# Windowed attention, MLP and routed experts in one kernel: the attention's tail reordered around MLP step 0, x of block 0 split from PSUM, filler matmuls from unit 10 on

## The reference, cut to what matters

```python
def _attn_ref(q, k, v, mem_k, mem_v):          # B=4, H=8, S=768, D=64, 8 memory keys
    for c in range(nc):                        # chunks of 32 queries
        k_full = np.concatenate([mem_k, k_ctx], axis=2)   # 16 keys to the left, 8 to the right
        scores = scale * np.matmul(q_c, k_full.transpose(0, 1, 3, 2))
        scores = scores - np.max(scores, axis=-1, keepdims=True)
        a = np.exp(scores)
        a = a / (np.sum(a, axis=-1, keepdims=True) + 1e-09)
        out[:, :, c_start:c_end] = np.matmul(a, v_full)

def _moe_ref(x, w_in, w_out, a, b):            # x 3072x512, w_in 512x2048, w_out 2048x512
    h = x @ w_in
    P = a[0] + a[1] * h + a[2] * h**2 + a[3] * h**3
    Q = 1.0 + np.abs(b[0]) * np.abs(h) + np.abs(b[1]) * h**2
    return (P / (Q + 1e-6)) @ w_out

def _moe2_ref(x, w_gate, w1, w2):              # 8 experts, each token goes to its best one
    ...
```

## Time and profile before

| | |
|---|---|
| three runs, median (lowest to highest) | 1076.66 us (1076.14 to 1079.69) |
| profiled execution | 1077.24 us |
| its span in the profile | 1075.4 us |
| mean granted TensorE clock | 0.976 of full speed |
| PE busy | 1013.0 us, 94% |
| DVE busy | 673.4 us, 63% |
| ACT busy | 589.9 us, 55% |
| POOL busy | 385.7 us, 36% |
| chain that ended last, by engine | PE 80%, DVE 8%, ACT 6%, issue 3%, DMA 2%, POOL 1% |

### The profile page before, as it was taken

The page is one execution under the profiler, slowest core; times in us unless marked ns, Lnnn a source line. Parts: engine busy times, 40 slices in busy tenths (PEclk is TensorE's granted clock), DMA queues, the critical chain, the costliest instruction groups (busy, mean ns, idle before and its releaser), DMA issues.

```text
span 1075.4 us, 20448 instructions
## 1 busy us (share of the span) xinstructions
PE 1013.0 (94%) x6272; PEld 834.9 (78%) x6273; DVE 673.4 (63%) x1327; ACT 589.9 (55%) x1256; POOL 385.7 (36%) x367
## 2 busy tenths in 40 slices
PE   8888889999999999999999999739999999999996
PEld 5767778888888888888888878527888888888885
DVE  6776788768867977887797778655225254322221
ACT  7876788766676666667667656605215144212121
POOL 2575344443444444344334434421212222212111
PEclk9998899999999999999999999959999999999999
DMA  8999500100010001001000120218115141111100
GB/s 315 386 407 353 221 1 21 33 27 20 0 59 0 20 0 59 20 0 59 0 20 1 40 98 1 99 59 303 32 46 186 46 185 33 42 40 34 49 24 14
DMA packets 34142, 90.05 MB, mean 84 GB/s; under 512 B 4262, under 2 KB 10534, under 8 KB 34096
## 3 DMA queue, kind: packets, MB, share of 16 engines
q1 hardware_dynamic: 29536, 76.86, 19.6%
q0 software_dynamic: 4560, 12.59, 3.5%
HBM read 72.13 MB, written 19.66 MB: 85 GB/s over the span
## 4 chain that ended last, share of the span: by engine, by line
PE 80%; DVE 8%; ACT 6%; issue 3%; DMA 2%; POOL 1%; DVEq 0%; POOLq 0%; ACTq 0%; SPq 0%
PE PS L478 22%; PE PS L573 21%; PE PS L671 14%; PE PS L705 14%; ACT prob L745 2%; PE PS L691 2%; PE PS L597 2%; PE PS L529 1%; PE PS L656 1%; DMA attention_out_t<-out_t 1%; DVE PS L910 1%; PE PS L500 1%; PE PS L609 1%; DVE g_sb L964 1%; DVE den L959 1%
## 5 line engine op out<-in xcount | busy, mean ns | idle before, releaser
L478 PE MATMUL PS<-xs,weights 128*128 (+1 forms) x1152 | 287.9, 399 | 0.0
L478 PEld LDWEIGHTS PS<-xs,weights 128*128 128x128 f32 x1152 | 215.5, 190 | 44.2
L573 PE MATMUL PS<-weights,g_hi 128*128 128x512 f32 x768 | 238.0, 391 | 6.1 <-POOL g_lo L1222 3.2
L1222 POOL TENSOR_TENSOR g_lo<-g_sb,g_hi 128x512 fp32r<-128x512 f32 x96 | 124.5, 1297 | 331.1 <-ACT g_hi L792 323.6
L573 PEld LDWEIGHTS PS<-weights,g_hi 128*128 128x128 f32 x768 | 143.5, 188 | 39.1 <-POOL g_lo L1222 6.3
L573 PE MATMUL PS<-weights,g_lo 128*128 128x512 f32 x384 | 149.6, 389 | 0.0
L671 PE MATMUL PS<-weights,xg_hi 128*128 x448 | 141.8, 398 | 3.1 <-DVE xg_lo L1155 2.6
L775 ACT ACTIVATE b_ln<-PS,cf 128x512 f32<-128x512 f32 x96 | 66.1, 689 | 128.2 <-PE PS L478 128.2
L705 PE MATMUL PS<-weights,h_hi 128*128 x432 | 135.8, 395 | 0.7 <-DVE weights L1032 0.7
L1225 POOL TENSOR_TENSOR den<-den,b_r 128x512 f32<-128x512 f32 x96 | 124.2, 1294 | 6.0 <-ACT b_r L798 6.0
L1155 DVE TENSOR_TENSOR xg_lo<-PS,xg_hi 128x512 fp32r<-128x512 f32 x29 | 20.0, 690 | 141.9 <-ACT xg_hi L815 141.9
(11 more groups left out here) (206 smaller groups left out, 1634.6 us busy)
## 6 DMA issues: line engine op xcount, KB each, us to landing
e_raw<-w_exp SPq DMA_DIRECT2D x35, 512.0 KB, 6.5
qk<-qk_all SPq DMA_DIRECT2D x32, 480.0 KB, 8.3
vw<-v_all SPq DMA_DIRECT2D x32, 384.0 KB, 8.0
w_raw<-w_mlp SPq DMA_DIRECT2D x16, 512.0 KB, 8.9
attention_out_t<-out_t SPq DMA_DIRECT2D x16, 384.0 KB, 7.2
x_raw<-attention_out_t SPq DMA_DIRECT2D x12, 512.0 KB, 5.0
mlp_out<-x SPq DMA_DIRECT2D x6, 1024.0 KB, 5.1
x_raw<-w_exp SPq DMA_DIRECT2D x5, 512.0 KB, 3.4
```

The costliest lines, as they stand in the source:

```text
L478: last = pe.matmul(PS[:, H_BANK + f % 2, :], w[:, wp], rhs, start=k == 0, stop=k == 3 * KT - 1)
L573: last = pe.matmul(PS[:, ACC_BANK + s, :], gp[:, f % 2, s * P:(s + 1) * P], w[:, wp], start=f == 0 and k == 0, stop=f == FT - 1 and k == 2)
L1222: pool.tensor_tensor(g_lo[:, q], g_sb[:], g_hi[:, q].bitcast(F32), ALU.subtract).then_inc(g_lo_done, 1)
```

## The change

1. *x of block 0 from PSUM.* For units 0 to 7 ACT writes the part of the output that belongs to the first 512 tokens directly into `xs` as `hi`: all 384 columns of an even unit, 128 of an odd one. The remaining 256 columns of the odd unit go to `out_t` as before. DVE subtracts `hi` from the PSUM bank to get `lo` (`lower_first`). PE's V of unit `u` waits for that (`first_lo_done`) as well, since both use the bank. The stores of pairs 0 to 3 shrink from 768 to 256 columns, the two loads of x for block 0 and POOL's four splits are gone.
2. *Weights.* POOL splits five pieces, after units 9, 13, 17, 21 and 25, where it split four after 11, 15, 21 and 27. Each load and each split in the steps moves accordingly; the piece that was split in step 7 is now split in step 6.
3. *Seam.* H of step 0 moves to iteration 31, H of step 1 to iteration 34. DVE does both of its last copies of transposed probabilities in step 0, ACT copies outputs 28 and 29 in step 0 and 30 and 31 in step 1. L580 moves from step 0 to step 4.
4. *Fillers.* From unit 10 on PE issues one matmul on zeros (128x384) ahead of each V.
5. The splits of x for the later blocks stand in steps 8, 10, 12 and 14, where they stood in 6, 8, 10 and 12.

```diff
-W_LOAD = {8: (0,), 12: (1,), 18: (2,), 22: (3,), 28: (4,), 30: (5,), 31: (6, 7), 32: (8, 9), 33: (10, 11), 34: (12, 13), 35: (14, 15)}
-W_POOL = {11: 0, 15: 1, 21: 2, 27: 3}
-W_STEP = {0: 4, 1: 5, 2: 6, 3: 7, 4: 8, 5: 9, 6: 10, 7: 11, 8: 12, 9: 13, 11: 14, 13: 15}
+W_LOAD = {6: (0,), 10: (1,), 14: (2,), 18: (3,), 22: (4,), 29: (5,), 30: (6,), 31: (7, 8), 32: (9, 10), 33: (11, 12), 34: (13, 14),
+          35: (15,)}
+W_POOL = {9: 0, 13: 1, 17: 2, 21: 3, 25: 4}
+W_STEP = {0: 5, 1: 6, 2: 7, 3: 8, 4: 9, 5: 10, 6: 11, 7: 12, 9: 13, 11: 14, 13: 15}
-H_EARLY = {32: 0, 33: 1}
+H_EARLY = {31: 0, 34: 1}
+STEADY_FROM = 10
+DIRECT = 8
-STEADY = 0
+STEADY = 1
...
+        def copies(u):
+
+            return (u + 1) // 2 if u < DIRECT else u + 1 - DIRECT // 2
...
@@ PE, unit loop
                     if u >= 2:
-                        pe.wait_ge(out_t_copied, u - 1)
-                    warm(STEADY, 6 + u % 2)
+                        if u - 2 < DIRECT:
+                            pe.wait_ge(first_lo_done, u - 1)
+                        if u > 2:
+                            pe.wait_ge(out_t_copied, copies(u - 2))
+                    if u >= STEADY_FROM:
+                        warm(STEADY, 6 + u % 2)
...
@@ ACT, copy_out
+                p, lo, hi = u // 2, (u % 2) * HALF, (u % 2 + 1) * HALF
                 act.wait_ge(out_t_ready, u + 1)
+                if u < DIRECT:
+                    act.activation(xs[:, p, lo:min(hi, TB)], PS[:, 6 + u % 2, 0:min(hi, TB) - lo], ACT.Copy).then_inc(first_hi_done, 1)
+                    if u % 2 == 0:
+                        return
+                    lo = TB
...
@@ DVE
+            def lower_first(u):
+
+                at = slice((u % 2) * HALF, min((u % 2 + 1) * HALF, TB))
+                dve.wait_ge(first_hi_done, u + 1)
+                if u % 2:
+                    dve.wait_ge(out_t_copied, copies(u))
+                dve.tensor_tensor(xs[:, KT + u // 2, at], PS[:, 6 + u % 2, 0:at.stop - at.start],
+                                  xs[:, u // 2, at].bitcast(F32), ALU.subtract).then_inc(first_lo_done, 1)
...
                 if d >= T_LAG:
                     copy_prob_t(d - T_LAG)
+                if 0 <= d - O_LAG < DIRECT:
+                    lower_first(d - O_LAG)
...
@@ DVE, step 0
-                if st.in_period(0) and st.m < 2:
-                    copy_prob_t(UNITS - 2 + st.m)
...
+                    if st.in_period(0) and st.m == 0:
+                        copy_prob_t(UNITS - 2)
...
+                    if st.in_period(0) and st.m == 0:
+                        copy_prob_t(UNITS - 1)
...
@@ POOL
-                for q in FIRST_SPLIT.get(u, ()):
-                    pool.wait_ge(x_in, 16 * (q // 2) + 16)
-                    pool.tensor_copy(x_quarter(0, 0, q, pool), raw_quarter(q)).then_inc(x_hi_done, 1)
-                    pool.wait_ge(x_hi_done, q + 1)
-                    pool.tensor_tensor(x_quarter(1, 0, q, pool), raw_quarter(q), x_quarter(0, 0, q, pool).bitcast(F32),
-                                       ALU.subtract).then_inc(x_lo_done, 1)
...
-X_SPLIT = (6, 8, 10, 12)
-X_LOAD = (16, 23)
-FIRST_SPLIT = {18: (0,), 19: (1,), 24: (2,), 25: (3,)}
+X_SPLIT = (8, 10, 12, 14)
```

More of the change, by code:

```diff
@@ L353, in load_x_half @@
         def load_x_half(sp, b, part):
-            if due(XQ * b + 2 * part):
-                sp.wait_ge(x_lo_done, XQ * b + 2 * part)
+            if due(XQ * (b - 1) + 2 * part):
+                sp.wait_ge(x_lo_done, XQ * (b - 1) + 2 * part)
             j = 2 * b + part
@@ L412, in _ @@
                     p = (d - O_LAG) // 2
[L413 to L419, removed]
+                    sp.wait_ge(out_t_copied, copies(2 * p + 1))
+                    at = TB if 2 * p < DIRECT else 0
+                    sp.dma_start(xt_dram[p][:, at:], out_t[:, p % 2, at:]).then_inc(out_t_stored[p % 2], 16)
                 for n in W_LOAD.get(d, ()):
@@ L566, in _ @@
                     if st.in_period(0) and f % 2 == 0:
-                        pe.wait_ge(late_lo_done, late(WCH + f // 2))
+                        if late(WCH + f // 2) > 0:
+                            pe.wait_ge(late_lo_done, late(WCH + f // 2))
+                        else:
+                            pe.wait_ge(w_lo_done, W_ORDER.index(WCH + f // 2) + 1)
                     if due(st.at(-1)):
@@ L575, in _ @@
                     last.then_inc(w2_done, 1)
-                if st.in_period(0) and st.m == 0:
-                    pe.wait_ge(out_t_copied, UNITS)
+                if st.in_period(0) and st.m == 4:
+                    pe.wait_ge(out_t_copied, copies(UNITS - 1))
                     pe.wait_ge(gate_in, 16)
@@ L730, in copy_out @@
             def copy_out(u):
+                p, lo, hi = u // 2, (u % 2) * HALF, (u % 2 + 1) * HALF
                 act.wait_ge(out_t_ready, u + 1)
+                if u < DIRECT:
[3 more added lines that the diff above has]
+                    lo = TB
                 if u >= 4:
-                    act.wait_ge(out_t_stored[u // 2 % 2], 16 * (u // 4))
-                act.activation(out_t[:, u // 2 % 2, (u % 2) * HALF:(u % 2 + 1) * HALF], PS[:, 6 + u % 2, 0:HALF],
-                               ACT.Copy).then_inc(out_t_copied, 1)
+                    act.wait_ge(out_t_stored[p % 2], 16 * (p // 2))
+                act.activation(out_t[:, p % 2, lo:hi], PS[:, 6 + u % 2, HALF - (hi - lo):HALF], ACT.Copy).then_inc(out_t_copied, 1)
             for d in range(UNITS + 1):
@@ L782, in _ @@
                                    bias=neg_a[:, 2:3]).then_inc(u_done, 1)
-                if st.in_period(0) and st.m < 2:
-                    for u in range(UNITS - 4 + 2 * st.m, UNITS - 2 + 2 * st.m):
-                        copy_out(u)
+                if st.in_period(0) and st.m == 0:
+                    copy_out(UNITS - 4)
+                    copy_out(UNITS - 3)
+                if st.in_period(0) and st.m == 1:
+                    copy_out(UNITS - 2)
                 if st.has(-1):
@@ L792, in _ @@
                     act.activation(g_hi[:, (st.m - 1) % 2], g_sb[:], ACT.Copy).then_inc(g_hi_done, 1)
+                if st.in_period(0) and st.m == 1:
+                    copy_out(UNITS - 1)
                 if st.has(0):
```

11 lines of the change are left out of this document (6 added, 5 removed).

## The result

The changed kernel takes 1083.4 us (median of 6 runs, 1081.49 to 1087.56) against 1077.74 (6 runs, 1076.14 to 1079.69) for the kernel before on the same chip: 5.7 us more, ratio 1.0057, 95% interval 1.0034 to 1.0080. Slower by more than 0.3%, as forecast (1082.3). The profiled execution took 1081.49 us, 4.25 more than that of before.

The account below looks back on a forecast made before the run. No engine was taken as full in the attention; a two-unit chain through DVE, ACT and PE bound it, PE later. Terms 13.4 + 0.5 - 3.1 + 1.0 - 6.2 = +5.6 gave 1082.3 us, range 1074.5 to 1090.

Parts of the forecast that it names:

- Term A: Units 0 to 7 through DVE: DVE and ACT take turns, +13.4 us, plus +0.5 for POOL's split beside them.
- Term B: Units 13 to 31: fewer loads, stores and POOL splits end stalls, less the fillers' cost; net -3.1 us.
- I give these 4.6 back: Units 21 to 23 and 27 to 29: stalls of 1.09 and 3.49 us over the usual pace expected to go.
- The fillers, +1.5: Matmuls ahead of V, 0.18 us each, on the two-unit chain in units 13 to 31: +1.5 us.
- Clock behind the slow stretch: PE idling in the slow units lowers its clock, costing less than one unit at that level behind them: +1.0 us.
- The rival that it would outlive the stretch: Six units behind unit 13 at the lower clock: +8.6 instead of +1.0, 1089.9 us; chance 0.13.
- Term C: Seam between attention and steps: earlier H and weights ready for W2 of step 8, -6.2 us.
- From step 9 on: Later steps: nothing changes, since PE is the bound and x's splits at 8 to 14 have slack.
- relief: Units 13 to 31: a full queue held the stretch, so all 8.7 us return; sum +0.5, 1077.2 us; chance 0.17.

Follow-up runs that it names:

- e1: Changed kernel with DVE's `lower_first` issued one iteration later, behind the next unit's bias: 1075.15 us, ratio 0.9975 to the kernel before.
- e2: Changed kernel with ACT's copy-out of unit d-5 ahead of the six exponentials of unit d instead of behind them: 1069.01 us, ratio 0.9922 to the kernel before.
- e8: e5 with GpSimd work put back where its four splits of x stood, on a buffer of ones, without transfers: 1086.59 us.
- e9: e5 with four loads of 512 KB put back, in iterations 8, 12, 16 and 23: 1087.53 us.
- e11: e5 with both put back, four loads of 512 KB and four GpSimd splits that wait for their loads: 1088.38 us.
- e12: e2 without fillers, with four loads of 512 KB and four GpSimd splits that wait for loads put back: 1071.60 us.
- e4: Changed kernel without the 22 filler matmuls ahead of V in units 10 to 31: 1083.29 us.
- e5: Kernel before with only x of block 0 taken straight from PSUM; no new weight tables, seam or fillers: 1086.55 us.
- e3: Changed kernel with x of block 0 through memory and split by POOL as before; the rest of the change kept: 1078.17 us.
- e6: Kernel before with one edit, ACT's copy-out of unit d-5 ahead of the exponentials of unit d: 1077.89 us.
- e10: Kernel before with GpSimd's splits of pieces 2 and 3 of x behind units 26 and 29 instead of 24 and 25: 1076.38 us.

## Why the prediction was right, and where it was not

- **Term A, 13.4 + 0.5: right, 13.2 for both, 0.7 less.** The steps of the turn were 4.36 and 4.18 (4.46 and 4.36 worked out), L931 0.56 and 0.29 us as estimated, DVE's wait 1.68 and 1.81 as named. One unit in eight, the one with POOL's split, takes 4.96 instead of 4.32: the +0.5 is there, as an L950 of 0.80 us. e1 and e2 show that it is the wait and not DVE's work: with the same work and no wait the eight units take 19.91 us, and the maxima need not stand behind ACT at all.
- **Term B, -3.1: measured -4.3; its size was off, and its reason for the most part wrong.** The step that failed is "I give these 4.6 back", put down to the splits and transfers gone. e8, e9 and e11 price these at 1 to 2 us behind a slow stretch; e12 shows 5.8 in a fast one. I had not asked whether the slow units would by themselves empty the queue in front of that stretch, though the sum had them giving the weight loads time. The fillers, +1.5, cost about 0.2 by the trace of e4.
- **Clock behind the slow stretch, +1.0: 0.** The clock did fall in it (0.66 in the window from 50) and cost nothing, since a turn leaves PE room; it was at 1.00 from 55 on. The rival that it would outlive the stretch falls: e5, without fillers, had 1.00 from 50 us on too. The Trainium skill (TensorE: Matmul & The Clock Gate, HAM oscillation — how this bites in real kernels) tells of a kernel whose idle gaps throttle the clock anew each time. The trace agrees in part: the clock fell more than once (0.85, 0.66), but it was at 1.00 from 40 to 50 us, in turns of the same kind.
- **Term C, -6.2: right, -6.27.** H of step 2 is back at 3.03, the piece for step 8 is in time, and g_lo, which ends at 160.06, lets W2 of step 8 go at 160.21, as worked out. e3 shows it without the direct x, 53.46.
- **From step 9 on, 0: +0.7, and +0.4 at the experts.** The prediction had PE as the bound from there, with slack for x's splits. PE's weight loads wait for g_lo in every second step (0.41, 0.26, 0.25 and 0.27 us), so that a step takes 5.51 us ((198.95 - 165.89)/6, the starts of W2) instead of 5.44. Before, with splits of weights and x in turn as well, they had no such wait: PE had lost 2.91 us in step 8, and ACT waited for its H (6.2 us in the eight steps behind, now 0.7). By the traces, then, ACT and DVE with their splits are a little slower than PE, and the wait in step 8 had hidden it; no run tests this. The 0.4 was not followed up.

The sum over the terms, +5.6, met the medians' +5.7. Some of this is luck. In the spans, which differ by 4.0, term A was 0.7 too high, term B with its fillers and the clock 2.2 too high together, the start and the rest of the span 1.3 too low; and the medians differ by 1.4 more than the two profiled executions do (4.25). The sum of the rival "relief" leaves the +1.0 of the clock out without saying so: with it the rival stood at +1.5.

Of the port lock, the Trainium skill (SBUF — State Buffer, Who interferes with whom) says that a VectorE operation with at most one SBUF input, outside the two-port modes, does not contend with GpSimd. The trace agrees. These are the subtraction of a split and, inside its time, L931 and L950 of DVE in the same turn:

```profile
47.71 2.34 POOL L1233 TENSOR_TENSOR weights<-w_raw,weights 128x1024 fp32r<-128x1024 f32 x1
```

```profile
48.80 0.56 DVE L931 TENSOR_TENSOR xs<-PS,xs 128x384 fp32r<-128x384 f32 x1 [1.68 <-ACT xs L746]
49.28 0.80 DVE L950 TENSOR_SCALAR rsafe<-rsum 128x6 f32<-128x6 f32 x1
```

L931 takes the 0.56 us that it takes without a split beside it; L950 takes 0.80 instead of 0.16 and ends when the split does.

## What to carry to other kernels

Before an operation that reads one engine's result is put on a second engine, look at where the first engine's part stands in its own order: here it stood behind six exponentials, and the two engines took turns. Moving it in front of them was worth 14 us, while moving the second engine's part later gave 8 and made a new chain. An edit that relieves a full queue has no price of its own: nearly the same loads and splits cost 1.8 us behind a slow stretch and 4.5 in a fast loop. A table of places that was made for one variant (e3's weight splits) can collide in the next.

## What the runs showed that I had not expected

- In the slow units the clock changed between its levels (windows at 0.85, 1.00, 1.00 and 0.66) instead of staying at one, though the turns are alike. Ahead of the first fall, at 33 us, PE was busy 0.29, 0.54 and 0.38 us in three windows of one microsecond; the longest that its rows show it idle in the eight units is 1.52 us. That it is busy 4.07 and 4.12 of 5 us in the windows with the lower clock, and 2.49 and 2.87 in those at 1.00, is the same work at the two levels.
- Nearly the same wait for weights in step 8 was followed by full clock in some kernels and by the lower level in others: 2.91 us before and 2.93 in e6, with 5.57 and 5.58 us to the next W2; 2.94 to 2.98 in e5, e8, e9, e10 and e11, with 7.18 to 7.22. That is 1.6 us, in one trace of each, and it stands in the spans of these kernels, e10 among them, but in no column of the table. Why it fell in one and not in the other stays open.
- A filler has 0.32 us in the rows and takes 0.25 from its start to V's, yet 22 of them cost nothing that can be measured in the changed kernel (1083.4 and 1083.29).
